# Pair sums at the head's end, routing of a batch over four heads, a weight split one block up, and a full-height last transpose

## What is computed

```python
q_pool = q.reshape(B, H, S // 2, 2, D).mean(axis=3)          # B, H, S, D = 4, 8, 1152, 64
scores = (q_pool @ k.T) / sqrt(D)
x = softmax(scores) @ v                                      # -> (2304, 512)
# layer 1: tokens with x @ w_skip > 0 go to their top expert, the others keep x
y[mask] = gate_w * (relu(x[mask] @ w1[e]) @ w2[e]);  x = x + y
# layer 2: every token goes to its top expert; also scaled by a sigmoid output gate of that expert
out[mask] = gate_w * sigmoid(x @ w_output_gate)[e] * (relu(x[mask] @ w1[e]) @ w2[e])
```

## Time and profile before

| | us |
|---|---|
| median of 3 runs | 1184.76 (1183.57 to 1188.63) |
| profiled execution | 1183.79 |
| its span, first to last instruction | 1182.0 |
| TensorE busy | 1129.2 (96%) |
| VectorE busy | 759.1 (64%) |
| ScalarE busy | 539.9 (46%) |
| GpSimd busy | 436.9 (37%) |

### The profile page before, as it was taken

How to read it: one execution, slowest core, us unless ns; L and a number is a source line. 1 busy time by engine, 2 the same in 40 slices (tenths; PEclk the granted TensorE clock), 3 DMA queues, 4 the chain that set the end, 5 groups by cost and what they waited for, 6 DMA issues and landing times.

```text
span 1182.0 us, 22128 instructions
## 1 busy us (share of the span) xinstructions
PE 1129.2 (96%) x7821; PEld 932.6 (79%) x7821; DVE 759.1 (64%) x1710; ACT 539.9 (46%) x945; POOL 436.9 (37%) x335
## 2 busy tenths in 40 slices
PE   7999999999999999999968999999979999999996
PEld 5777677777777777677757899989869999999995
DVE  6667677776687676876345776776636655655551
ACT  3555555555555555555404444444224434344320
POOL 0766666677666776667830000000000000000100
PEclk9999999999999999999989999999889999999998
DMA  5262224233322332221166613174484453141100
GB/s 125 63 216 57 69 72 132 71 80 76 87 70 52 84 83 76 71 61 45 48 228 206 259 36 141 65 283 158 169 300 154 174 207 140 53 170 36 36 19 14
DMA packets 74398, 132.61 MB, mean 112 GB/s; under 512 B 11040, under 2 KB 29472, under 8 KB 74320
## 3 DMA queue, kind: packets, MB, share of 16 engines
q10 hardware_dynamic: 26240, 69.22, 16.1%
q1 hardware_dynamic: 43424, 50.58, 15.9%
q0 software_dynamic: 4656, 11.79, 2.9%
HBM read 106.12 MB, written 19.24 MB: 106 GB/s over the span
## 4 chain that ended last, share of the span: by engine, by line
PE 75%; DVE 15%; issue 3%; ACT 2%; DMA 2%; ACTq 1%; POOL 1%; DVEq 0%; SPq 0%; POOLq 0%
PE PS L724 19%; PE PS L575 9%; PE PS L545 7%; PE PS L491 7%; PE PS L558 6%; PE PS L741 6%; PE PS L737 6%; PE PS L738 5%; PE PS L559 5%; DVE mx L1027 4%; DVE W2L L1131 2%; DVE KA L1010 2%; DVE KA L1007 2%; DVE arena_a L1001 1%; PE PS L612 1%
## 5 line engine op out<-in xcount | busy, mean ns | idle before, releaser
L443 POOL TENSOR_TENSOR arena_a<-arena_a,arena_p 128x576 f32<-128x576 f32 x224 | 325.7, 1454 | 121.2 <-ACT arena_p L840 103.7
L1027 DVE TENSOR_REDUCE mx<-PS 128x1 f32<-128x384 f32 (+1 forms) x480 | 246.8, 551 | 139.6 <-PE PS L545 135.2
L724 PE MATMUL PS<-moe,W 128*128 128x128 f32 x2432 | 282.0, 277 | 2.8 <-ACT moe L926 2.8
L724 PEld LDWEIGHTS PS<-moe,W 128*128 128x128 f32 x2432 | 279.1, 194 | 5.2 <-ACT moe L926 3.5
L840 ACT ACTIVATE arena_p<-PS 128x576 f32<-128x576 f32 x288 | 187.3, 652 | 171.3 <-PE PS L559 165.5
L558 PE MATMUL PS<-QHT,KA 128*128 128x288 f32 x576 | 192.6, 338 | 0.5 <-ACT QLT L851 0.5
L545 PE MATMUL PS<-KA,QHT 128*128 128x384 f32 (+1 forms) x480 | 174.0, 363 | 11.7 <-DVE mx L1027 11.6
L1131 DVE TENSOR_TENSOR W2L<-W2R,W2H 128x1024 fp32r<-128x1024 f32 x148 | 171.3, 1217 | 1.6 <-ACT W2H L812 1.6
L559 PE MATMUL PS<-QLT,KB 65*128 65x288 f32 x576 | 169.2, 297 | 0.0
L812 ACT CAST W2H<-W2R 128x1024 fp32r<-128x1024 f32 x148 | 144.3, 1048 | 51.2 <-PE PS L741 40.3
L575 PE MATMUL PS<-arena_p,arena_a 128*64 128x288 f32 x1152 | 160.5, 414 | 0.0
(11 more groups left out here) (173 smaller groups left out, 1177.0 us busy)
## 6 DMA issues: line engine op xcount, KB each, us to landing
W<-in_moe_w ACTq DMA_DIRECT2D x16, 2048.0 KB, 14.2
W2R<-in_moe_w ACTq DMA_DIRECT2D x16, 2048.0 KB
moe<-xs SPq DMA_DIRECT2D x40, 258.0 KB, 2.7
arena_a<-in_k SPq DMA_DIRECT2D x32, 288.0 KB, 2.9
arena_a<-in_v SPq DMA_DIRECT2D x32, 288.0 KB, 2.8
KB<-KA SPq DMA_DIRECT2D x32, 288.0 KB
arena_a<-in_q SPq DMA_DIRECT2D x32, 256.0 KB, 3.2
xs<-padrow SPq DMA_DIRECT2D x8, 258.0 KB, 3.3
```

Of the source, the lines that this page charges most:

```text
L443: nc.gpsimd.tensor_tensor(Acc[u], Acc[u], P[u][:, t, :], ALU.add).then_inc(acc_step, 1)
L724: last = nc.tensor.matmul(PS[:, HB + f // 4, (f % 4) * PN:(f % 4 + 1) * PN], W1[s][:, d, f * PN:(f + 1) * PN], xT[:, d, :], start=(d == 0) ...
L1027: vec.reduce_max(mx3[0:n, t, c:c + 1], PS[0:n, MXB + b % 2, 0:KB_], AX.X).then_inc(pr_max, 1)
```

## The change

Four edits. `pool_q(h + 2)` is called at the start of VectorE's pass, before block 0, and no longer behind block 1. The routing's steps are spread over four passes in place of three, behind blocks 5 and 9 (and one behind `divide`) in place of 5, 10 and the end; with it `Rsum`'s reduction, `Racc`'s addition and the conversion to `Raccb` each move to a later step. `w2_low` in heads 3 to 6 stands behind block 9, not 10. `trans_qh` turns the last query tile with all its 128 rows, of which 64 hold queries.

```diff
-        RT_GAPS = {(0, 5): [0], (0, 10): [1, 2, 3], (0, NBLK): [4, 5], (1, 5): [6], (1, 10): [7], (1, NBLK): [8, 9],
-                   (2, 5): [10, 11], (2, 10): [12, 13, 14, 15], (2, NBLK): [16, 17]}
+        RT_GAPS = {(0, 5): [0], (0, 9): [1, 2, 3], (1, 5): [4, 5], (1, 9): [6, 7], (1, NBLK): [8], (2, 5): [9],
+                   (2, 9): [10], (3, 5): [11, 12], (3, 9): [13, 14, 15, 16, 17]}
...
                 for t in range(3 * j, min(QT, 3 * j + 3)):
-                    n = PN if t < QT - 1 else Q_LAST
                     o = (t % 3) * PN
-                    last = transpose(PS[:, TR, o:o + n], QN[0:n, t].rearrange("p f d -> p (f d)"), n)
+                    last = transpose(PS[:, TR, o:o + PN], QN[:, t].rearrange("p f d -> p (f d)"))
...
                 elif n == 6:
-                    vec.tensor_reduce(Rsum[:, :], R_b.rearrange("p t a e -> p (a e) t"), AX.X, ALU.add)
                     ins = vec.tensor_tensor(R[:, T, 0, :], gc_b[:, :, 1, :], L[:, T, 1 + 2 * E:NL], ALU.mult)
                 elif n == 7:
                     vec.tensor_reduce(osel[:, T], R[:, T, 0, :], AX.X, ALU.add).then_inc(rt_osel, 1)
-                    ins = vec.tensor_tensor(Racc[0:OP, :], Racc[0:OP, :], Rsum[:, :], ALU.add)
+                    ins = vec.tensor_reduce(Rsum[:, :], R_b.rearrange("p t a e -> p (a e) t"), AX.X, ALU.add)
...
                 elif n == 9:
+                    vec.tensor_tensor(Rf, Rf, R_b.rearrange("p t a e -> p t (a e)"), ALU.mult)
+                    ins = vec.tensor_tensor(Racc[0:OP, :], Racc[0:OP, :], Rsum[:, :], ALU.add)
+                elif n == 10:
                     vec.tensor_copy(Raccb[:, :], Racc[:, :]).then_inc(rt_acc, 1)
-                    ins = vec.tensor_tensor(Rf, Rf, R_b.rearrange("p t a e -> p t (a e)"), ALU.mult)
-                elif n == 10:
                     ins = vec.tensor_reduce(posf[:, T], Rf, AX.X, ALU.add)
...
-                routing = [(late, b) for b, at in enumerate(RANKS_IN) for late in range(3) if h == at + late]
+                routing = [(late, b) for b, at in enumerate(RANKS_IN) for late in range(4) if h == at + late]
...
+                if has(h + 2):
+                    pool_q(h + 2)
                 for b in range(NBLK):
                     if has(h + 1):
                         block_max(h + 1, b)
                     if has(h + 2):
                         if b == 1:
-                            pool_q(h + 2)
                             k_low(h + 2, 0)
...
-                    if h in SPLIT_IN and b == 10:
+                    if h in SPLIT_IN and b == 9:
                         w2_low(0, 0, 0, [SPLIT_IN.index(h)])
```

## The result

The changed kernel takes **1168.28 us** (median of 4 runs, 1167.38 to 1169.7) against 1184.9 of the kernel before in the same comparison: a ratio of 0.9856, 95% interval 0.9831 to 0.988. The forecast was 1168.0. The profiled execution took 1167.38, its span is 1165.6.

What follows compares the result with a forecast made beforehand. TensorE, busy 96% of the span, bounds the kernel, so the spacing of its work counts. -10.0 - 7.8 + 1.4 - 0.4 + 0.1 = -16.7 gave a forecast of 1168.0 us, with over 8 in 10 within 1161.5 to 1176.

Steps and rivals of the forecast that it cites:

- Part 1: Pair sum moved before block 0: TensorE's wait before block 4's weight load goes, 0.36 us in 28 heads, -10.0.
- the 0.12 that I had booked with the routing: Second routing head: pair sum ending 0.12 us later than in a plain head, a delay expected to go.
- Part 2: Last query tile transposed with 128 rows: the 64-row gap before the next matmul goes, 0.27 us in 29 heads, -7.8.
- The 0.02 a head that I took off for the maxima of blocks 6 and 7: Taken from the transpose's 0.29 us, as those maxima would end just where blocks 8 and 9's matmuls need them.
- Part 3: Weight split before block 10, four heads: subtraction waits for GpSimd's second addition, delay 1.21 us instead of 0.85, +1.4.
- The margin that decides it: Heads 3 to 6: ScalarE's copy ends 0.15 us too late for the subtraction to get ahead of GpSimd's second addition.
- Part 4: Routing over four heads: 0.53, 0.35, 0 and 0.53 over plain heads, 1.41 a batch, three batches, -0.4.
- Part 5: Last batch: conversion to Raccb some 0.35 us later, 0.25 covered, delaying the counting matmul: +0.1, at most 0.35.
- The 64-row gap staying: Rival: the gap at the last query transposes belongs to the place, not the shape; 1175.8 us, chance 8%.
- the wait coming back by half: Rival: k's copies or block 3 are late next, returning 0.18 us in 28 heads, +5; 1173 us, chance 9%.
- split and routing using the idle slot: Rival: both really use VectorE's idle slot, split -2.8 and routing about -2.4; 1162 us, chance 18%.
- GpSimd keeping the sum out for both additions: Rival: pair sum waits for both GpSimd additions, block 2 starts 0.94 us later in 28 heads; 1204 us, chance 3%.

Runs made afterwards that it cites:

- the turn alone: Kernel before, with only the last query tile's transpose changed to 128 rows: 1175.41 us, 8.24 less over heads 1 to 30.
- the pair sum alone: Kernel before, with only the pair sum moved to the head's start: 1173.09 us, 10.49 less over heads 1 to 30.
- the split put back: Changed kernel, with the weight split's low halves back behind block 10: 1164.91 us, 1.41 less over heads 1 to 30.
- its copy moved: Changed kernel, with ScalarE's rounding copy for the weight split issued one exponential earlier: 1161.77 us, 4.84 less over heads 1 to 30.
- mended twice: Kernel with early split copy and re-placed routing, step 6's wait dropped, fourth head's reciprocal and multiplication put ahead of conversion and index copy: 1157.41 us.
- both: Changed kernel, with the split's copy one exponential earlier and the routing steps re-placed around GpSimd's additions: 1160.59 us.
- routing in the gaps: Changed kernel, with routing steps re-placed to start before GpSimd's second addition: 1165.3 us, 0.44 less over heads 1 to 30.
- the old routing: Changed kernel, with a batch's routing over three heads in the old order: 1167.16 us, 0.19 less over heads 1 to 30.

## Why the prediction was right

**Part 1, the pair sum**: -10.0 forecast, -10.49 alone. The step was 1.35 - 0.99 = 0.36 a head, and plain heads gave 17.76 - 17.41 = 0.35. Most of the rest is that the second routing head of each batch gained 0.45 (18.23 to 17.78): the 0.12 that I had booked with the routing belongs here. I had left open who wins the ports at 310.5 and priced both at nothing. The traces have both: VectorE won in the plain heads (0.48 long, and GpSimd's pair 0.33 longer), and where step 8 of the routing stands ahead of the sum it lost and lasted 1.61 us, and that head is still 17.09.

**Part 2, the turn**: -7.8 forecast, -8.24 alone. The 0.02 a head that I took off for the maxima of blocks 6 and 7 was not needed. The row of three 128-row transposes beside the 64-row pair was the right thing to price it by. The rule on columns in the Trainium skill (TensorE: Matmul & The Clock Gate, "Back-to-back issue gap") would have had the edit cost 0.8 us, by the estimate above; the measurement goes the other way. It fits what the Trainium skill says elsewhere (TensorEngine Tiling (Array Packing), "Key Properties"), that a change of mode drains the engine. That the 0.29 us are such a drain no run here shows, only that they go with the 64-row shape.

**Part 3, the split**: +1.4 forecast, +1.41. Heads 3 to 6 are 18.33 against the 18.3 of the text, L1130 is 2.32 long and ends 1.08 behind the addition, where 1.09 was forecast. The margin that decides it, 0.15 us between copy and addition, was 0.17. The idle slot in front of block 10 was idle on VectorE alone.

**Part 4, the routing**: -0.4 forecast, +0.19 measured against the old order on the same kernel. This is the step that was off. First, the 0.12 of the second head was credited to the wrong part: it goes with part 1 whatever the routing does, and the fair base is 1.41 a batch and not 1.53. Second, the fourth head costs 0.62, not the 0.53 that I carried over from the first: six short operations stand in front of block 10 there, and not four, and block 10's maximum starts 12.39 us into the fourth head, 12.30 into the first. The first (0.51), second (0.35) and third head (-0.04) came as worked out.

**Part 5**: +0.1 forecast. The counting matmul's idle time grew from 1.97 to 2.27:

```profile
589.82 0.17 PE L705 MATMUL PS<-Raccb,onesb 128*1 128x16 bf16 x1 [2.27 <-DVE Raccb L1099]
```

What of this reaches the end was not tried; all behind head 31's start is 0.38 shorter, and that stretch differs by more than this between executions (602.12 and 601.52 in the two of the kernel after, 601.22 to 603.22 among the kernels here).

**The sum** over the heads was -16.8 by the steps and -17.11 by the trace. That the whole came out at -16.4 is two things I had not reckoned with: 1.09 us more at the start, made of a head 0 at half clock that is 2.1 longer and an attention that began 1.0 earlier, and the 0.38 less at the end. The agreement of the median with 1168.0 is a little luck: the same kernel gave 1166.13 the second time.

**The rivals.** The 64-row gap staying is out by the turn alone; the wait coming back by half, by the 0.99 of the pair sum alone; split and routing using the idle slot (18%), by the split put back and by its copy moved. GpSimd keeping the sum out for both additions never happened; and when the sum lost against one, nothing was late, so that rival needed both.

## What to carry to other kernels

A slot in which an engine is idle is not free if its operation needs something that another engine holds: here, ask for each elementwise VectorE operation from SBUF to SBUF which GpSimd instruction runs at its start, since starting 0.08 us behind one made an operation 1.2 us longer. Such a loss is mended by issuing the operation earlier, even into the middle of the addition before, or by dropping a wait it doesn't need; both together took 8.2 us off heads 1 to 30 here, where the change itself had taken 17.1. And the same edit has to be priced at each place it is made: ask what the engine waits for next.

## What the runs showed of the hardware

- A VectorE subtraction, addition or multiplication of two SBUF tensors, or a conversion from SBUF to SBUF, and a GpSimd addition exclude each other for whole instructions, also when it is tiny: a conversion of 96x6 elements took 1.36 us, a multiplication of 96x12 1.32, where 0.16 and 0.20 are usual. The VectorE operation then ends its own length less 0.13 us behind the addition (1.22 and 1.08). Subtractions and maxima that read PSUM kept their 0.69 and 0.55 beside additions. So did some operations from SBUF to SBUF: a reduction of 96x48 to 96x6 took 0.20 us both inside an addition (203.88 us, mended twice) and outside one (205.08 us, both), and the reciprocal of 96x6 took its usual 0.19 inside one (302.51 us, after). The Trainium skill (SBUF — State Buffer, "SBUF: two separate sides") has the rule that the first keeps the ports for the whole instruction, and the traces agree: in the heads of all kernels here, each operation of the first kind whose start is recorded in a running addition, more than 13 ns behind its start, ended behind that addition. In the rows above, the additions that had to wait came out 0.33 to 0.80 us longer.
- Within those 13 ns the recorded starts don't decide: a multiplication recorded 9 ns behind GpSimd's second addition lost (1.46 us long), a pair sum recorded 1 ns behind the first, or up to 13 ns in another kernel (routing in the gaps, 371.31 us), won (0.48).
- A 64-row transpose among 128-row ones cost TensorE 0.29 us more than a 128-row one (8.24 us over heads 1 to 30), and 0.26 at the head's last transposes (0.73 in place of 0.47).
- In the heads the granted clock was at its lower level of 1.2 GHz in stretches that differ in place and length between executions of one kernel: 3.4 us in head 0 in one, 6.8 us in heads 5 and 6 in the other. TensorE was busy in the whole 2 us ahead of the fall at 126 us, and for 0.84 of the 2 us before those. The first cost 2.4 us, the second 2.8; in the kernels with the split put back and the old routing a stretch of 3.4 us began at the start of head 0 and cost about 1.2 (15.6 in place of 14.4).
